# An fp32 weight product among attention's slots, with idle transposes of the identity in the first four

## What is computed

```python
# attention: B=2, H=8, S=768, D=64; block 32, window 16
k_sum = k.reshape(B, H, nb, block, D).max(axis=3)
v_sum = v.reshape(B, H, nb, block, D).mean(axis=3)
scores = [where(|i-j| < 16, scale*q@k.T, -1e9) , scale*q@k_sum.T + log(32)]
x = softmax(scores) @ [v, v_sum]                 # then to (B, S, 512)
# block 2: w_in 512x1024, w_spatial 768x768, w_out 512x512
h = relu(x @ w_in); u, v = halves of h; v_n = layer norm of v
g = u * (w_spatial @ v_n + b_spatial)
y = g @ w_out
# block 3: moe2_w_in 512x1024, conv of 3 taps along S, moe2_w_out 1024x512
h = relu(y @ moe2_w_in)
out = (h * sigmoid(conv(h))) @ moe2_w_out
```

## Time and profile before

| | |
|---|---|
| median of 3 runs | 368.81 us (368.1 to 368.98) |
| the profiled execution's own time | 368.71 us |
| its span | 366.9 us |
| TensorE matmul busy | 338.2 us (92%) |
| VectorE, ScalarE, GpSimd busy | 213.1, 127.0, 115.5 us |
| mean granted TensorE clock | 0.94 |
| moved by DMA | 30.53 MB, 83 GB/s over the span |

### The profile page before, as it was taken

How to read it: one execution, slowest core, us unless ns; L and a number is a source line. 1 busy time by engine, 2 the same in 40 slices (tenths; PEclk the granted TensorE clock), 3 DMA queues, 4 the chain that set the end, 5 groups by cost and what they waited for, 6 DMA issues and landing times.

```text
span 366.9 us, 5885 instructions
## 1 busy us (share of the span) xinstructions
PE 338.2 (92%) x2288; PEld 295.8 (81%) x2288; DVE 213.1 (58%) x498; ACT 127.0 (35%) x364; POOL 115.5 (31%) x116
## 2 busy tenths in 40 slices
PE   4577685998998999999999999999999999999996
PEld 4355464676788889988999999999999888889984
DVE  1757576445330599235444697588855667756662
ACT  1555756655652414334211112422312213221111
POOL 3477767654230699960000591000000000000000
PEclk9557858699999999999999999999999999999999
DMA  7996885464000121015400010000000003000004
GB/s 307 324 330 207 277 277 166 125 217 145 2 3 0 45 100 43 2 41 185 119 0 2 4 54 2 1 2 0 0 2 0 0 2 145 27 2 0 2 1 172
DMA packets 9275, 30.53 MB, mean 83 GB/s; under 512 B 1184, under 2 KB 1184, under 8 KB 9248
## 3 DMA queue, kind: packets, MB, share of 16 engines
q1 hardware_dynamic: 9104, 29.77, 24.1%
q10 hardware_dynamic: 144, 0.39, 0.3%
HBM read 27.01 MB, written 3.15 MB: 82 GB/s over the span
## 4 chain that ended last, share of the span: by engine, by line
PE 79%; ACT 8%; DMA 5%; DVE 4%; issue 3%; POOL 0%; DVEq 0%; POOLq 0%
PE bank L756 25%; PE bank L758 25%; PE bank L757 24%; ACT P L470 6%; DMA kw<-in_kw 4%; PE bank L748 2%; PE bank L735 2%; ACT pT L465 1%; DVE P L601 1%; DVE x_l L577 1%; ACT x_h L459 1%; PE bank L725 1%; DVE rinv L584 1%; DMA out<-obuf 1%; DVE ks L541 1%
## 5 line engine op out<-in xcount | busy, mean ns | idle before, releaser
L470 ACT ACTIVATE P<-P,nmax 128x120 f32<-128x120 f32 x96 | 36.7, 383 | 38.7 <-DVE nmax L601 38.7
L758 PE MATMUL bank<-g_h,W_l 128*128 128x384 f32 x128 | 43.0, 336 | 0.0
L757 PE MATMUL bank<-g_l,W_h 128*128 128x384 f32 x128 | 42.9, 335 | 0.0
L756 PE MATMUL bank<-g_h,W_h 128*128 128x384 f32 x128 | 42.9, 335 | 0.0
L577 DVE TENSOR_TENSOR x_l<-bank,x_h 128x256 fp32r<-128x256 f32 x24 | 10.2, 425 | 52.1 <-ACT x_h L459 52.1
L757 PE MATMUL bank<-wo_l,hg_h 128*128 128x512 f32 x96 | 38.0, 396 | 0.0
L758 PE MATMUL bank<-wo_h,hg_l 128*128 128x512 f32 x96 | 38.0, 396 | 0.0
L756 PE MATMUL bank<-wo_h,hg_h 128*128 128x512 f32 x96 | 37.9, 395 | 0.0
L383 POOL TENSOR_TENSOR P<-P,rinv 128x480 f32<-128x480 f32 x24 | 23.7, 987 | 42.0 <-DVE rinv L586 42.0
L758 PE MATMUL bank<-wsT_h,vn_l 128*128 128x384 f32 x96 | 32.1, 334 | 0.0
L756 PE MATMUL bank<-wsT_h,vn_h 128*128 128x384 f32 x96 | 32.1, 334 | 0.0
(11 more groups left out here) (96 smaller groups left out, 778.0 us busy)
## 6 DMA issues: line engine op xcount, KB each, us to landing
kw<-in_kw SPq DMA_DIRECT2D x8, 720.0 KB, 4.3
vw<-in_vw SPq DMA_DIRECT2D x8, 576.0 KB, 5.3
vT<-in_vT SPq DMA_DIRECT2D x8, 384.0 KB, 6.4
out<-obuf SPq DMA_DIRECT2D x12, 256.0 KB, 2.1
qT<-in_q SPq DMA_DIRECT2D x7, 384.0 KB, 5.1
stage<-in_wsT SPq DMA_DIRECT2D x6, 384.0 KB, 2.8
stage<-in_w_in SPq DMA_DIRECT2D x4, 512.0 KB, 10.8
stage<-in_w SPq DMA_DIRECT2D x4, 512.0 KB, 4.9
```

Source lines behind the costliest of these rows:

```text
L470: a.activation(P[:, i % NP_, j, :], P[:, i % NP_, j, :], ACT.Exp, bias=nmax[:, c:c + 1], scale=-1.0, accum_out=rsum[:, c:c + 1]).then_inc( ...
L756: t_.matmul(dst, lhs[0](c), rhs[0](c), start=first, stop=False)
L757: t_.matmul(dst, lhs[0](c), rhs[1](c), start=False, stop=False)
L758: ins = t_.matmul(dst, lhs[1](c), rhs[0](c), start=False, stop=last)
```

## The change

The weight product is made in plain fp32 from unsplit weights: one matmul for each of 4 chunks of 8 units, 32 in all, in the place of 96 fp32r matmuls. These 32 pieces are put among attention's slots, three in each of slots 4 to 11 and two in each of slots 12 to 15. `woT` and `w2` are loaded whole, straight into the space of `x1`, early in SyncE's queue. ScalarE takes a finished unit at the end of its slot, VectorE subtracts in the next slot (`low_W`). The first dense product moves from slots 16 to 27 to slots 17 to 28. `values` gets two banks in turn, the ring of the fills three instead of four, and `x_l` is made one slot later. The value sums are spread by a DMA (`load_sums`) instead of GpSimd. Key loads are issued in two halves, and the first query load goes behind them in SyncE's queue. Twenty instead of sixteen transposes come ahead of the first scores, and eight transposes of the identity (`KEEP`) into each of slots 0 to 3, whose results nobody reads. The six `wsT` chunks are split in a row when the last u unit is done. The rest of the layout in SBUF follows from this.

```diff
-    WARM = 16
-    SLOTS = NG + 4
+    WARM, KEEP = 20, 8
+    SLOTS = NG + 5
...
-        SC, PTB, OT = bank[4:6], bank[6], bank[7]
+        SC, PTB, OT = bank[4:6], bank[6], [bank[3], bank[7]]
...
+        pieces = [(("W", f, n), c, c + 1) for n in range(2) for f in range(FC) for c in range(KC)]
+        for i in range(4, 16):
+            for _ in range(3 if i < 12 else 2):
+                fills_at[i].append(pieces.pop(0))
         b0 = [("v", 0, m) for m in range(SC6)] + [("u", 0, f, n) for f in range(FC) for n in range(2)]
-        for n, i in enumerate((16, 17, 18, 19, 20, 21, 22, 23, 24, 24, 25, 25, 26, 27)):
-            fills_at[i].append(b0[n])
+        for n, i in enumerate((17, 18, 19, 20, 21, 22, 23, 24, 24, 25, 25, 26, 27, 28)):
+            fills_at[i].append((b0[n], 0, KC))
...
-        seq += [("W", f, n) for n in range(2) for f in range(FC)]
...
-            return n % 4 if n < ATT else (4 + n - ATT) % 8
+            return n % 3 if n < ATT else (4 + n - ATT) % 8
...
-                sp.dma_start(kw[:, p % 2, :, :], kw_in[p]).then_inc(k_in[p % 2], 16)
+                for h in range(2):
+                    tiles = slice(h * NT // 2, (h + 1) * NT // 2)
+                    sp.dma_start(kw[:, p % 2, tiles, :], kw_in[p, :, tiles, :]).then_inc(k_in[p % 2], 16)
...
+            def load_sums(p):
+
+                sp.wait_ge(vsum_ready, p + 1)
+                if p >= NVB:
+                    sp.wait_ge(pv_done, GP * (p - NVB + 1))
+                sp.dma_start(vw[KW:KA, p % NVB, :, :],
+                             vsum[KW:KA, p % 2, :].unsqueeze(1).to_broadcast([NB, NT, 2 * D])).then_inc(vw_ready[p % 2], 16)
...
             load_k(0)
+            load_q(0)
             load_vT(0)
             load_k(1)
+            load_vT(1)
+            load_v(0)
             load_q(1)
+            sp.dma_start(woT[:, :, :], woT_in.rearrange("p (c m) -> p c m", c=KC)).then_inc(wo_in, 16)
+            sp.dma_start(w2[:, 0, :, :], w_in2[0].rearrange("p (c m) -> p c m", c=KC)).then_inc(w2_in[0], 16)
+            load_sums(0)
+            load_k(2)
             load_item(0)
...
-                if u[0] == "W" and n - SC6 - 2 * FC < SC6:
-                    c = n - SC6 - 2 * FC
-                    stage_wait(act, ("ws", c))
-                    a.activation(wsT_h[c][:, :], stage[:, item[("ws", c)] % NST, 0:S], ACT.Copy).then_inc(wsh_ready, 1)
+
+            for c in range(SC6):
+                stage_wait(act, ("ws", c))
+                a.activation(wsT_h[c][:, :], stage[:, item[("ws", c)] % NST, 0:S], ACT.Copy).then_inc(wsh_ready, 1)
...
+            for c in range(SC6):
+                if c == 0:
+                    dve.wait_ge(ring_done, done_count(("u", 1, FC - 1, 1)))
+                dve.wait_ge(wsh_ready, c + 1)
+                vv.tensor_tensor(out=wsT_l[c][:, :], in0=stage[:, item["ws", c] % NST, 0:S],
+                                 in1=wsT_h[c][:, :].bitcast(fp32), op=ALU.subtract).then_inc(wsl_ready, 1)
...
-                    ins = three(bk[:, :], range(KC),
-                                [lambda c: woT_h[:, c, col], lambda c: woT_l[:, c, col]],
-                                [lambda c: w2_h[:, c, cg], lambda c: w2_l[:, c, cg]])
+                    col = slice(f * 128, (f + 1) * 128)
+                    for c in range(lo, hi):
+                        ins = t_.matmul(bk[:, :], woT[:, c, col], w2[:, n, c, :], start=(c == 0), stop=(c == KC - 1))
...
+                if i < 4:
+                    for _ in range(KEEP):
+                        t_.transpose(bank[1][:, 0:128], ident[:, :], ident[:, :])
```

More of the change, by code:

```diff
@@ L82, in overlay @@
             return found
[L84 to L88, removed]
+        W_h, W_l = sb("W_h", [128, FC, FF], f32r), sb("W_l", [128, FC, FF], f32r)
         wi_h, wi_l, *ws_most, hbuf, cbuf, hg_h, hg_l = overlay(
@@ L340, in split_part @@
                 nonlocal n_hi
[L341 to L349 removed]
+                c, cols = x[1], slice((part - 1) * 512, part * 512)
                 if part == 0:
@@ L472, in _ @@
                                      accum_out=rsum[:, c:c + 1]).then_inc(exp_done, 1)
-                for u in fills_at[i]:
-                    take(u)
+                for u, _, last in fills_at[i]:
+                    if last == KC:
+                        take(u)
             def v_std(t):
@@ L562, in v_norm, with low_W @@
                                  ALU.subtract, ALU.mult).then_inc(vn_ready, 1)
+            def low_W(u):
+                _, f, n = u
+                at = n * FC + f
+                cols = slice(n * 512, (n + 1) * 512)
+                dve.wait_ge(Wh_ready, at + 1)
+                vv.tensor_tensor(out=W_l[:, f, cols], in0=bank[bank_no(place[u])][:, :],
+                                 in1=W_h[:, f, cols].bitcast(fp32), op=ALU.subtract).then_inc(Wl_ready, 1)
             key_maxima(0)
@@ L622, in _ @@
                     v_norm(t - 1)
-            for n in range(2):
-                for f in range(FC):
-                    at = n * FC + f
-                    cols = slice(n * 512, (n + 1) * 512)
-                    dve.wait_ge(Wh_ready, at + 1)
-                    src = bank[bank_no(place["W", f, n])]
-                    vv.tensor_tensor(out=W_l[:, f, cols], in0=src[:, :], in1=W_h[:, f, cols].bitcast(fp32),
-                                     op=ALU.subtract).then_inc(Wl_ready, 1)
-                    if at < SC6:
-                        dve.wait_ge(wsh_ready, at + 1)
-                        vv.tensor_tensor(out=wsT_l[at][:, :], in0=stage[:, item["ws", at] % NST, 0:S],
-                                         in1=wsT_h[at][:, :].bitcast(fp32), op=ALU.subtract).then_inc(wsl_ready, 1)
+            for c in range(SC6):
[4 more added lines that the diff above has]
+                                 in1=wsT_h[c][:, :].bitcast(fp32), op=ALU.subtract).then_inc(wsl_ready, 1)
             def out_of_ring(u):
@@ L779, in dense @@
                 bk = bank[bank_no(n)]
-                if before_it[n] is not None:
+                if before_it[n] is not None and lo == 0:
                     pe.wait_ge(*before_it[n])
```

194 lines of the change are left out of this document (86 added, 108 removed).

## The result

The changed kernel takes **372.01 us** (median of 4 runs, 371.62 to 375.0) beside 368.77 us for the kernel before (4 runs, 368.1 to 368.98): ratio 1.0109, 95% interval 1.0055 to 1.0162, slower. Run once more as a control beside the experiments, it stood at 1.0186 (1.0109 to 1.0264). Where some executions of a kernel were in a slower state (one of the control's, four of experiment 4's, one of the first in experiment 6), median and ratio are of the others. The forecast was 367.0 us; the result lies at the upper end of its range (372.0), and on the other side of no change.

A forecast was written before the change was run, and what follows sets the result against it. Waits on other engines and loads bound the head, TensorE the dense stretches behind 69.59 us. From 368.7: +8.8 to the last u unit, -21.8 product stretch, +9.0 gap, +2.2 clock, giving 367.0 us; range 363.5 to 372.

The forecast's parts named there:

- the head up to slot 5: Slots 0 to 4: fewer bytes ahead of pair 2's key load, -1.3 us; first piece of slot 5 at 26.9.
- The 0.4 us for longer rows: In the head's loads: a guessed saving of 0.4 us for fewer, longer rows, 8 KB each in the weights.
- rival 2: Head queue late through the value sums, or ScalarE and VectorE pace eight slots: 8 x 0.3 or 2.5; 369.5 us; chance 0.13.
- A slot over 5.3: Sign in the changed profile that the forecast is wrong; slots 5 to 11 were expected at 5.0 us.
- The gap: TensorE idle behind the last u unit while `wsT` chunks are split and reloaded: +9.0 us, bounds 8 and 11.
- The clock behind the gap: After the idle gap the clock drops to half and half that time is lost: +2.2 us, bounds 0 and 3.2.
- The slots' chain: Slots 5 to 16: 5.0 us with three pieces, 4.1 with two; first dense unit at 81.0, +11.4 us.
- 0.88 a piece: Price of one fp32 matmul of 512 columns in the slots: 0.88 us, between 0.68 and 1.32.
- Half as the slots' growth: Of the 21.8 us saved, nearly all comes back: half as longer slots, half as the bared split.
- Rival 1: In the head, idle transposes leave the clock at half until real work comes: +4.9 us, 371.9 us; chance 0.20.
- Rival 3: Cheaper gap behind the u units: loads land in 1.8 us, clock returns at once; 363.8 us; chance 0.13.
- rival 4: A piece costs 1.32 us, over 29 pieces in slots 5 to 15: +12.8 us, 379.8 us; chance 0.03.

The follow-up runs named there:

- experiment 4: The change, with chunks 0 to 4 of `wsT` split during the last u units, only chunk 5 behind them: 362.65 us, 0.9845 of the kernel before.
- experiment 6: Four kernels: the change with a quarter of the pieces, 365.89 us; with relieved queue, quarter pieces 362.38, quarter pieces and operand loads 357.74, all pieces and quarter loads 366.25.
- experiment 3: The change, with the value sums spread by GpSimd and the second half of `w2` loaded behind the keys of pair 3: 367.4 us, 1.0006 of the kernel before.
- experiment 2: Four kernels against the change: second half of `w2` behind pair 3's keys, 371.17 us; first sums copy from ScalarE's queue, 373.7; both, 372.43; sums by GpSimd, 373.32.
- experiment 1: The change without the eight idle transposes in each of slots 0 to 3, the twenty ahead of the first scores kept: 374.93 us, 1.0207 of the kernel before.
- the last kernel above: The change with sums by GpSimd, `w2`'s second half behind pair 3's keys, five `wsT` chunks split ahead, and no idle transposes between scores: 358.42 us, 0.976.

## Why the prediction was wrong

*The step that failed* is the first: the head up to slot 5 (-1.3 us, bounds -2.5 and +1), and that behind it no slot waits for the queue. "About 0.3 MB less lies ahead of the key load for pair 2": that load landed at 22.4, as forecast (22.8). (The totals, 6.6 and 6.9 MB, are right; the list beside them leaves out a third `w_in` chunk and a `vT`. The 0.4 us for longer rows stayed a guess that no run tests.) But the text went by the keys alone. The copy of the value sums was given a bound of +1 us through SyncE's wait, and rival 2 had "one wait of 2.5" for it, with a chance of 0.13. It became the wait of slot 3 (4.13 us). "The three pieces of slot 4 lie ahead of it, in the wait for the keys" did not come true either: they start at 23.91, behind the landing. So the first piece of slot 5 stood at 28.89 instead of 26.9: +2.0. And nothing was asked of the next pair's keys: the load of pair 3 now stood behind half of `w2`, a `w_in` chunk and the copies, and cost two slots (6.25 and 6.32 us instead of 5.0; the other five took 4.87): +1.9. Together 3.7 with the small terms. A slot over 5.3 was one of the forecast's own signs of being wrong.

This division is that of one profile. In the two others of the same head the first piece of slot 5 is 3.9 and 5.6 us late, with a clock that had fallen behind the wait for the sums, and slots 7 and 8 take 9.9 and 10.5 us together instead of 12.6. The two waits cover each other in part, which is why removing one brought nothing and removing both gave 81.28, and a time equal to the kernel before.

*The gap* was sized too small: 10.8 instead of 9.0. The landing of 2.8 us was the median of loads that were spread out. With three issued at once the page of after has a median of 4.6 for the six, and the last of the three was ready 6.5 us after the first issue. That was the upper bound ("11 (in 4)"). The reading itself held: with the chunks split ahead, 8.7 us come back, and the clock with them.

*The clock behind the gap* held (1.7 of 2.2).

*The slots' chain* held in its numbers: 0.88 a piece, 4.87 for 5.0, 3.9 to 4.1 for two pieces, slots 15 and 16 together 6.79 for 6.75. What it meant was only half right. "Half as the slots' growth" reads as if the pieces cost that; with three quarters of them gone only 5 to 7 us come back, since under them lie the waits for the loads, 3 MB of which the product brought into the head itself.

*Rival 1 was wrong.* The clock was up within slot 0, in TensorE's timeline of the change (L816 are the idle transposes, eight of which took 1.09 us; L721 the scores, 0.64 at full clock as against 1.08 in the earlier trace rows):

```profile
1.54 4.53 PE L808 MATMUL bank<-ident 128*128 128x128 f32 x20 [1.54 <-POOL ident L333]
6.31 0.96 PE L721 MATMUL bank<-kw,qT 64*64 64x120 f32 x16 [0.24 <-POOL kw L373]
7.21 1.09 PE L816 MATMUL bank<-ident 128*128 128x128 f32 x8
8.31 0.64 PE L721 MATMUL bank<-kw,qT 64*64 64x120 f32 x16
```

The rule of the Trainium skill that was weighed there ("TensorE: Matmul & The Clock Gate", Part 4: PE-mode transpose) says that such work does not count as busy for the gate in the same way; the traces here do not agree. In the change twenty transposes took 4.53 us, all at half pace, and the clock rose during the scores right behind them (0.96, between 1.08 and 0.64). In the kernel of experiment 3 it rose while nothing but transposes had run, since the same twenty took less:

```profile
1.54 3.91 PE L814 MATMUL bank<-ident 128*128 128x128 f32 x20 [1.54 <-POOL ident L323]
```

Rival 1's time, 371.9, came out all the same, for another reason. So did its picture of slot 4 in the control (pieces from 24.53 at half clock, slot 5 at 30.77; the rival had 24.7 and 31.8): there the clock had been up, and fell behind the wait for the sums. A hit by such a number proves nothing.

*Rival 3* had the sign of the gap's error wrong; *rival 4* fell with the 0.88.

## What to carry to other kernels

Where work is moved ahead, move its operands' bytes in the sum too: list every load that the head's slots wait for, those of the new operands too, not only the one that is critical now, and ask of each what is newly ahead of it in the queue. A delay that was the last to end may hide another of the same size, so that two edits can be worth nothing singly and all of the loss together; one profile then shows only one of the ways in which the loss can be divided. And when a stretch is taken out, look at once at what it covered: here the useful part of the change came only with the splits moved ahead, 2.6% under the kernel before instead of 1 to 2% over it.

## What the hardware showed that was not expected

- A copy of 144 KB in rows of 512 bytes took 8 to 10 us beside large loads, in SyncE's queue as in ScalarE's, and once 18 us (the second copy in the kernel with a quarter of the pieces). That it is slower by its small rows was not tried apart.
- A load's landing depends on what is issued near it: the key load of pair 3, 720 KB in two, took 5.6 to 14.5 us from its second issue in the runs above. With half of `w2` issued behind it, it was 6.8 and 5.6 in experiment 2, but 9.3 in experiment 3; and issued 2.8 us earlier, with all of `w2` ahead, it landed no earlier.
- The column of the granted clock reads 1.00 ahead of its first recorded change, whatever the pace. In experiment 1 it reads so up to 24 us, while the scores up to there take 1.08 us, the half-clock time. The duration of a known instruction tells it.
- The clock rose in twenty transposes or right behind them, and fell again without more of them: with none between the scores, those of slot 0 took 0.64 us and those of slot 1 1.08, behind an idle 1.01 us, in the last kernel above. With eight transposes between them, the scores of the change still took 0.64 behind an idle 1.11 us.
- It does not always rise: in experiment 1 the twenty took 4.53 us, 1.73 idle us followed, and the scores of slot 0 took 1.08.
